# Attention front end: P·V of the first 16 steps from whole 32-bit floats, and every normalising step there on GpSimd

## The reference

```python
scores = scale * np.matmul(q, k.transpose(0, 1, 3, 2))
thresh = np.max(scores, axis=-1, keepdims=True) - tau
scores = np.where(scores >= thresh, scores, -1000000000.0)
scores = scores - np.max(scores, axis=-1, keepdims=True)
attn = np.exp(scores)
attn = attn / (np.sum(attn, axis=-1, keepdims=True) + 1e-09)
attn_out = np.matmul(attn, v)
...
h = x @ w_in
x = (h * (1.0 / (1.0 + np.exp(-1.702 * h)))) @ w_out
...
h = x @ w_in2
sp = np.where(h > 20.0, h, np.log1p(np.exp(np.minimum(h, 20.0))))
out = (h * np.tanh(sp)) @ w_out2
```

## Time and profile before

| | us |
|---|---|
| median of 3 runs | 1164.22 |
| range of the runs | 1163.97 to 1164.56 |
| the profiled execution's own time | 1164.77 |
| its span, first to last instruction | 1163.0 |
| PE busy | 1102.5 (95%) |
| DVE busy | 774.3 (67%) |
| ACT busy | 738.7 (64%) |
| POOL busy | 315.8 (27%) |

### The profile page before, as it was taken

One profiled execution on the slowest core, in us unless ns is written; L12 is line 12 of the kernel. 1 busy time (PEld: TensorE's weight loads), 2 busy tenths in 40 slices (PEclk: granted clock), 3 DMA queues, 4 the chain that ended last, 5 costly groups with the idle time before them and its releaser, 6 DMA issues.

```text
span 1163.0 us, 19459 instructions
## 1 busy us (share of the span) xinstructions
PE 1102.5 (95%) x7472; PEld 1037.8 (89%) x7472; DVE 774.3 (67%) x1383; ACT 738.7 (64%) x1019; POOL 315.8 (27%) x526
## 2 busy tenths in 40 slices
PE   6678889999999999999999999999999999999998
PEld 5568889998999999999999999998999989899997
DVE  6978788888888888888888533665433444344343
ACT  6878787867777777778767322467545554554453
POOL 6876674434444433344333000000000000000000
PEclk9879999999999999999999999999999999999999
DMA  4443524232143222233231003520010000000000
GB/s 123 138 133 114 162 81 111 60 94 82 50 109 94 60 85 76 73 108 85 65 106 30 25 19 104 190 79 28 4 51 1 28 28 28 28 28 28 1 28 27
DMA packets 93948, 80.43 MB, mean 69 GB/s; under 512 B 47520, under 2 KB 79264, under 8 KB 93856
## 3 DMA queue, kind: packets, MB, share of 16 engines
q1 hardware_dynamic: 93856, 79.19, 23.4%
HBM read 65.54 MB, written 13.63 MB: 68 GB/s over the span
## 4 chain that ended last, share of the span: by engine, by line
PE 74%; DVE 13%; ACT 7%; issue 4%; POOL 0%; DMA 0%; ACTq 0%; DVEq 0%
PE ps_s L693 17%; PE ps_r L577 13%; PE ps_r L598 11%; PE ps_r L716 9%; PE ps_t L449 5%; PE ps_t L463 5%; PE ps_t L716 4%; PE ps_s L436 4%; PE ps_t L598 3%; DVE pt_lo L519 2%; DVE neg_max L499 2%; DVE x_pair L533 2%; ACT pv_half_sb L495 2%; DVE e_buf L506 2%; DVE q_st L400 2%
## 5 line engine op out<-in xcount | busy, mean ns | idle before, releaser
L577 PE MATMUL ps_r<-x_hi,wi_lo 128*128 128x256 f32 x544 | 158.7, 292 | 1.9 <-DVE x_lo L651 1.9
L760 DVE COPY hidden<-ps_s 128x768 f32<-128x768 f32 x48 | 45.8, 956 | 170.5 <-PE ps_s L693 170.5
L449 PE MATMUL ps_t<-ident,e_buf 128*128 128x128 f32 x720 | 118.8, 285 | 38.6 <-DVE pt_lo L519 27.5
L577 PE MATMUL ps_r<-x_lo,wi_hi 128*128 128x256 f32 x544 | 154.4, 284 | 0.0
L577 PE MATMUL ps_r<-x_hi,wi_hi 128*128 128x256 f32 x544 | 154.4, 284 | 0.0
L487 ACT CAST pt_hi<-ps_t 128x640 fp32r<-128x640 f32 x144 | 100.1, 695 | 82.7 <-PE ps_t L449 80.2
L789 ACT ACTIVATE m_lo_raw<-m_lo_raw 128x1536 f32<-128x1536 f32 x24 | 35.8, 1491 | 168.8 <-DVE m_lo_raw L767 168.8
L449 PEld LDWEIGHTS ps_t<-ident,e_buf 128*128 128x128 f32 x720 | 85.9, 144 | 58.9 <-issue 29.6
L598 PE MATMUL ps_r<-g_hi,wo_lo 128*128 128x256 f32 x464 | 135.3, 292 | 0.0
L693 PE MATMUL ps_s<-x_hi,wi_lo 128*128 128x384 f32 x384 | 129.0, 336 | 2.4 <-DVE x_lo L749 2.4
L598 PE MATMUL ps_r<-g_lo,wo_hi 128*128 128x256 f32 x464 | 130.9, 282 | 0.0
(11 more groups left out here) (100 smaller groups left out, 3058.1 us busy)
## 6 DMA issues: line engine op xcount, KB each, us to landing
k_ll_raw<-in_k SPq DMA_DIRECT2D x64, 288.0 KB, 2.9
v_st_raw<-in_v SPq DMA_DIRECT2D x64, 160.0 KB, 2.9
wi_lo_raw<-in_moe_w_in SPq DMA_DIRECT2D x16, 512.0 KB, 3.8
wo_lo_raw<-in_moe_w_out SPq DMA_DIRECT2D x16, 512.0 KB, 4.4
q_raw<-in_q SPq DMA_DIRECT2D x32, 192.0 KB, 2.9
x_scratch<-y_acc SPq DMA_DIRECT2D x9, 512.0 KB, 3.3
x_lo_raw<-x_scratch SPq DMA_DIRECT2D x6, 768.0 KB, 4.7
out_rows<-rows_out SPq DMA_DIRECT2D x18, 256.0 KB, 2.1
```

The source lines that it names most:

```text
L449: mm = pe.transpose(t_flat[:, j * P:(j + 1) * P], e_buf[n % 3][:, j * P:(j + 1) * P], ident[:, :])
L577: mm = pe.matmul(bank[:, part * CH:(part + 1) * CH], wi[w][:, k, f * P:(f + 1) * P], x[:, k, :], start=t == 0, stop=t == 3 * KT - 1)
```

## The change

In the 16 steps of the front, and there alone:

- P·V is made from whole floats: `pe_pv` takes `v_raw` (64 columns) as it comes from memory and `pt_raw` or `pt2_raw`, the turned weights copied out whole. That is one matmul for each key tile, 5 for a group, with 64 output rows.
- So the rounding of V (L407), its rest (L412), the rest of the turned weights (L519), and the copy and sum of two halves (L495, L533) are gone for these groups. ACT still copies the turned weights out of PSUM, as whole floats.
- A new `act_x_first` copies the group's result straight to `x_raw`; it stands in ACT's step n for the group that ended with n-3, one step earlier than `act_pv` did, at even n.
- The turn of n+1 waits for the copy (`p_hi`) of n alone.
- All 16 rows are normalised on POOL, at POOL's place for normalising: ahead of the row operations of the next step.
- The rounding of the first chunk's input moves one step earlier for its first three quarters.

```diff
-            if n < FRONT and (n // 2) % 2 == 1:
+            if n < FRONT:
                 cols = slice((n % 2) * P, (n % 2 + 1) * P)
-                return pt2_hi[:, :, cols], pt2_lo[:, :, cols]
+                return ((pt_raw, pt2_raw)[(n // 2) % 2][:, :, cols],)
...
                 if normed_by_pool(n):
-                    pe.wait_ge(s["normed_even"], n // 2 + 1)
+                    pe.wait_ge(s["normed_first"], n + 1)
...
-                if n >= 1:
-                    pe.wait_ge(s["p_lo"], n)
+                if 1 <= n <= FRONT:
+                    pe.wait_ge(s["p_hi"], n)
+                elif n > FRONT:
+                    pe.wait_ge(s["p_lo"], n - FRONT)
...
+            if g < H:
+                pe.wait_ge(s["p_hi"], last + 1)
+                pe.wait_ge(v_in[u % 2], 16 * (u // 2 + 1))
+                if g >= 2:
+                    wait_sums(pe, g - 1)
+                v, out_rows = v_raw[u % 2][:, :, D:P], slice(0, D)
...
             for j in range(NJ):
-                for part, pt in enumerate((lo, hi)):
-                    mm = pe.matmul(pv_bank(g)[:, 0:w], v_st[u % 2][:, j, :], pt[:, j, :],
-                                   start=j == 0 and part == 0, stop=j == NJ - 1 and part == 1)
+                for part, pt in enumerate(parts):
+                    mm = pe.matmul(pv_bank(g)[out_rows, 0:w], v[:, j, :], pt[:, j, :],
+                                   start=j == 0 and part == 0, stop=j == NJ - 1 and part == len(parts) - 1)
...
         def normed_by_pool(n):
 
-            return n < FRONT and n % 2 == 0
+            return n < FRONT
...
+        def act_x_first(act, g):
+            h = GROUPS[g][1]
+            base = (h % 2) * D
+            act.wait_ge(s["pv_done"], g + 1)
+            act.copy(x_raw[base:base + D, h // 2, 0:256], pv_bank(g)[0:D, 0:256]).then_inc(s["x_first"], 1)
...
-                turn_first = n < FRONT + 2 or n - 3 not in GROUP_AT
+                turn_first = n < FRONT + 3 or n - 3 not in GROUP_AT
...
-                if n < FRONT + 2 and n - 4 in GROUP_AT:
-                    act_pv(act, GROUP_AT[n - 4])
+                if n < FRONT + 3 and n - 3 in GROUP_AT:
+                    act_x_first(act, GROUP_AT[n - 3])
...
-                if 0 <= n - 2 < N:
+                if FRONT <= n - 2 < N:
                     dve_p_lo(dve, n - 2)
-                if n < FRONT + 2 and n - 4 in GROUP_AT:
-                    dve_pv(dve, GROUP_AT[n - 4])
```

More of the change, by code:

```diff
@@ L205, in thresholded_attention_two_mlps @@
         pv_half_sb = cut("att", "pv_half_sb", 320, dt=F32)
-        pt2_hi = place("pt2_hi", [NJ, 256], F32R, at["mlp"])
+        pt2_raw = place("pt2_raw", [NJ, 256], F32, at["mlp"])
         g_hi = cut("mlp", "g_hi", 8 * CH)
-        pt2_lo = place("pt2_lo", [NJ, 256], F32R, at["mlp"])
         g_lo, gated = cut_both("mlp", "g_lo", 8 * CH)
@@ L278, in pv_moving @@
         def pv_moving(g):
-            if g < H and g % 2 == 1:
-                return pt2_hi[:, :, 0:256], pt2_lo[:, :, 0:256]
+            if g < H:
+                return ((pt_raw, pt2_raw)[g % 2][:, :, 0:256],)
             lo, w = group_cols(g)
-            return pt_hi[:, :, lo:lo + w], pt_lo[:, :, lo:lo + w]
+            return pt_lo[:, :, lo:lo + w], pt_hi[:, :, lo:lo + w]
         def x1_place(g):
@@ L304, in x1_count, with wait_sums @@
             return sum(len(x1_stores(x)) for x in range(g) if x1_place(x) == place)
+        def wait_sums(engine, count):
+            if count <= H:
+                engine.wait_ge(s["x_first"], count)
+            else:
+                engine.wait_ge(s["pv_sum"], count - H)
         def pv_bank(g):
@@ L322, in ring_release @@
             if m in (0, 1):
-                pe.wait_ge(s["p_lo"], N)
-                pe.wait_ge(s["pv_sum"], len(GROUPS))
+                pe.wait_ge(s["p_lo"], N - FRONT)
+                wait_sums(pe, len(GROUPS))
                 return
             if k < 2:
-                pe.wait_ge(s["pv_sum"], H)
+                wait_sums(pe, H)
                 return
@@ L418, in thresholded_attention_two_mlps @@
             for table, at_ in ((KQ_PREP, first - 3), (Q_LO, first - 2), (V_PREP, first + 2)):
-                table.setdefault(max(at_, -1), []).append(u)
+                if u >= H or table is not V_PREP:
+                    table.setdefault(max(at_, -1), []).append(u)
         def pe_scores(pe, n):
@@ L454, in pe_pv @@
             _, _, _, u, last = GROUPS[g]
-            pe.wait_ge(s["p_lo"], last + 1)
-            pe.wait_ge(s["v_lo"], u + 1)
-            if g >= 2:
-                pe.wait_ge(s["pv_sum"], g - 1 if g < H else g)
-            hi, lo = pv_moving(g)
-            w = group_cols(g)[1]
+            w = group_cols(g)[1]
+            if g < H:
+                pe.wait_ge(s["p_hi"], last + 1)
[3 more added lines that the diff above has]
+                v, out_rows = v_raw[u % 2][:, :, D:P], slice(0, D)
+            else:
+                pe.wait_ge(s["p_lo"], last + 1 - FRONT)
+                pe.wait_ge(s["v_lo"], u - H + 1)
+                wait_sums(pe, g)
+                v, out_rows = v_st[u % 2], slice(0, P)
+            parts = pv_moving(g)
             for j in range(NJ):
-                for part, pt in enumerate((lo, hi)):
-                    mm = pe.matmul(pv_bank(g)[:, 0:w], v_st[u % 2][:, j, :], pt[:, j, :],
-                                   start=j == 0 and part == 0, stop=j == NJ - 1 and part == 1)
+                for part, pt in enumerate(parts):
+                    mm = pe.matmul(pv_bank(g)[out_rows, 0:w], v[:, j, :], pt[:, j, :],
+                                   start=j == 0 and part == 0, stop=j == NJ - 1 and part == len(parts) - 1)
             mm.then_inc(s["pv_done"], 1)
@@ L525, in dve_pv @@
             par, grp = x1_place(g)
-            dve.wait_ge(s["pv_half"], g + 1)
-            if g < H:
-                rows = x_raw[base:base + D, h // 2, 0:w]
-            else:
-                rows = x_pair[base:base + D, grp * 256:grp * 256 + w]
-                if x1_count(g, (par, grp)):
-                    dve.wait_ge(x1_out[par][grp], 16 * x1_count(g, (par, grp)))
+            rows = x_pair[base:base + D, grp * 256:grp * 256 + w]
+            dve.wait_ge(s["pv_half"], g - H + 1)
+            if x1_count(g, (par, grp)):
+                dve.wait_ge(x1_out[par][grp], 16 * x1_count(g, (par, grp)))
             dve.tensor_tensor(rows, pv_bank(g)[0:D, 0:w], pv_half_sb[base:base + D, 0:w], ALU.add).then_inc(
@@ L674, in thresholded_attention_two_mlps @@
         X_HI = {slot - 2: c for c, slot in START_SLOT.items() if c >= 1}
-        X_HI_FIRST = {max(GROUPS[2 * k + 1][4] + 4, 0) if k < KT - 1 else GROUPS[2 * k + 1][4] + 3: k for k in range(KT)}
+        X_HI_FIRST = {GROUPS[2 * k + 1][4] + 3: k for k in range(KT)}
         def pe_up2(pe, g):
@@ L902, in _ @@
                     act_g_hi(act, pair)
-                if n >= FRONT + 2 and n - 3 in GROUP_AT:
+                if n >= FRONT + 3 and n - 3 in GROUP_AT:
                     act_pv(act, GROUP_AT[n - 3])
@@ L1056, in groups_summed @@
         def groups_summed(n):
-            return [GROUP_AT[m] for m in ([n - 4] if n < FRONT + 2 else [n - 3]) if m in GROUP_AT]
+            return [GROUP_AT[n - 3]] if n >= FRONT + 3 and n - 3 in GROUP_AT else []
         @block.sync
@@ L1101, in _ @@
                 if k == ALONE[-12]:
-                    sp.wait_ge(s["p_lo"], N)
+                    sp.wait_ge(s["p_lo"], N - FRONT)
                     sp.wait_ge(s["pv_done"], len(GROUPS))
```

21 lines of the change are left out of this document (10 added, 11 removed).

## The result

| | before | after |
|---|---|---|
| median of 9 runs, us | 1164.56 | 1166.93 |
| range of the runs | 1163.97 to 1166.56 | 1166.79 to 1171.55 |
| span of the profiled execution | 1163.0 | 1165.1 |
| mean granted clock over the span | 0.991 | 0.994 |

The changed kernel takes 1.0025 times as long as the one before (95% interval 1.0014 to 1.0036): 2.4 us slower by the medians, 2.9 by this ratio. The interval leaves out 1, so it is slower, if only by a quarter of a per cent.

The account below looks back on a forecast made before the run. Ahead of the first MLP matmul, chains through engines in fixed order set the pace; PE bounds from 85 us on. Front +0.4, step 18 +0.4, clock +2.5: +3.3 on 1164.77 is 1168.1, less 0.55 gives 1167.5 (range 1161.5 to 1172.5).

Parts of the forecast that it names:

- Product of whole floats, 2.4: P·V of a group on PE at full clock: between 1.2 and 2.4 us, taken as 2.4 (four partial products).
- Ring A: Two front steps, odd exp through mask, scores, group product (V), turn and copy-out to exp: 3.82 + V = 6.2 us.
- Ring B: Two front steps through POOL's rest of K, normalising and threshold, then mask, max, exp: 6.2 us, 7.5 with a weight piece.
- The exps up to step 15: Starts of exp at odd steps 5 to 15 of the front: from 24.4 to 60.3 us.
- Exp of 15 to exp of 17: End of the front: late mask, product, then copy, weights, copy-out and normalising of 16 take 8.7 us, to 69.0.
- The chain of step 18: From exp of 17 to the first chunk's last rounding: 7.5 us for 7.1 before, +0.4.
- The clock, two 3.4 us stretches at 1.25: PE's falls to 1.2 GHz ahead of the MLP: two stretches costing 1.25 us each, +2.5, with 0 and 6 as ends.
- Turns that wait for PE's own queue: Sign expected in the trace of after: the front's turns wait for PE's own queue, no longer for `p_lo`.
- The clock holds: Rival: longer products keep PE's clock up, or it falls once off the chain; +0.8 ± 1.5, about 1165.0; chance 0.27.
- The product is cheap: Rival: a group's product takes 1.2 us, so POOL's ring alone decides; about 1161; chance 0.18 together with light POOL.
- Light POOL: Rival: POOL's queue binds less than worked out, DVE being free, so faster; chance 0.18 together with the cheap product.
- Low clock each time: Rival: every group product meets the low clock and takes 4.3 us, about +1.5 for each of six pairs; 1174; chance 0.10.

Follow-up runs that it names:

- whole_fill: The changed kernel with idle PE matmuls added, 4 in each odd step from 5 to 17 and 8 in step 19: 1165.13 us, ratio 1.0005.
- odd_on_act: The changed kernel with the front's odd rows normalised on ACT again, even rows on POOL: 1165.17 us, ratio 1.0000.
- odd_on_act_fill: The changed kernel with odd rows on ACT again and idle PE matmuls, 4 per odd step 5 to 17, 8 in step 19: 1162.73 us, ratio 0.9982.

## Why the prediction came out as it did

The forecast, 1167.5 against 1166.93, rests on the right mechanisms; some of its sizes were off and partly made up for one another. That it is only 0.6 off is in part luck: it added 3.3 us, and 2.4 were measured (2.1 on the span), but the kernel before came out 0.34 higher in the runs that after is compared with (1164.56 for 1164.22).

- *What bounds the kernel, and that only the first MLP matmul counts.* Right: shift there 2.03, shift of the span 2.1.
- *Product of whole floats, 2.4.* Right side of a range of 1.2 to 2.4; measured 2.16 for one more, 2.30 from its start to the turn's.
- *Ring A, 3.82 + V.* Right: 6.20 in after, 6.10 without its rival, 8.24 with two products.
- *Ring B, 6.2 plain, 7.5 to 8.0 with weights.* Right: 6.19 and 6.20 where the product is short; 8.33 and 7.43 in the pairs from 9 to 13, for 8.0 and 7.5 (and 7.06 from 13 to 15, for 7.3 through the product). One term was too small, the normalising: 0.97 from its start to the threshold's, where the 0.79 of before was taken. That the two would tie was in the numbers.
- *Up to exp of step 3 nothing binds differently, 16.6.* The number is right (16.62) by luck, the sentence isn't: the mask of step 2 waited 1.07 for POOL's threshold, and without the odd rows on POOL that exp comes at 16.21.
- *The exps up to step 15*, 24.4, 30.6, 37.5, 45.5, 53.0, 60.3, against 23.73, 29.93, 36.52, 44.85, 52.28, 59.34. The mis-sized term is the first product, which meets the clock's rise: I gave it 3.5 us (19.4 to 22.9), with the rise at 21.9 as in before, and the turn behind it started 2.81 after it (19.53 to 22.34), since the clock rose sooner, near 20.6 (its weight loads are 0.42 apart at 20.02 and 20.44, and then there are seven within 1.51); so all later exps are 0.7 early. Step 8 was 0.3 shorter yet. The front was therefore not 0.3 behind before at step 15, as worked out, but 0.7 ahead.
- *Exp of 15 to exp of 17, 8.7 with the clock held.* 8.49 in `whole_fill`.
- *The chain of step 18, +0.4.* It came as +0.15.
- *The clock, two 3.4 us stretches at 1.25.* Size right by luck (2.55 from `whole_fill` to after at the exp of step 17, against 2.5), form wrong: one stretch of 6.8 us on one product.
- *The sum.* Predicted 0.4 for the front, 0.4 for the chain of step 18 and 2.5 for the clock, 3.3; measured -0.67 (67.96 against 68.63), +0.15 and +2.55, 2.03. Of the 1.04 by which the front came earlier than worked out (67.96 for 69.0), 0.54 are the first product's term (23.86 for 24.4 in `whole_fill`), 0.29 lie from there to step 15, and 0.21 from 15 to 17; the chain of step 18 makes 0.25 more.
- *"If the clock's falls go away" the prediction is wrong.* They did not; they became fewer. After has two (61.6 and 78.6, 6.8 us each), before four (20.5 us in all).
- *"Turns that wait for PE's own queue."* Only in part: 7 turns waited 7.6 us in all for the row from POOL, the longest 2.5.
- *Rivals.* "The clock holds" did not happen by itself. `whole_fill` is near it, and its 1165.13 is near the 1165.0 named, but with the idle matmuls' own cost in it. "The product is cheap" fell with V = 2.2. "Light POOL" fell: DVE waited 11 times for the threshold, 14.1 us. "Low clock each time" fell: one product of eight ran all through at half clock.

What stays open is why a fall comes at group 6 in after, `odd_on_act` and `odd_on_act_fill`. The rows show that PE had been busy for 0.8 to 1.7 of the 3.4 us ahead, but such stretches occur elsewhere in these kernels (1.07 of 3.40 from 36.0 us in after, with no fall behind it), and I have no rule for which of them count.
